# Gated attention and two expert layers: the second quarter's alpha, keys and queries loaded as rows of twelve tokens and transposed by VectorE

## The reference

```
# q, k, v, alpha: batch 2, 8 heads, 768 tokens, 48 columns
for t in range(S):
    state = alpha[:, :, t, :, None] * state + einsum('bhd,bhde', k[:, :, t], v[:, :, t])
    y[:, :, t] = einsum('bhd,bhde->bhe', q[:, :, t], state)
# x = y as 1536 tokens x 384
xn = x / sqrt(mean(x*x) + 1e-6) * rms_g
x  = (silu(xn @ w_gate) * (xn @ w_val)) @ w_out            # 384 -> 1536 -> 384
p  = probs / (sum(probs) + 1e-9)                           # 4 experts
out = sum_e p[:, e] * (relu(x @ w1[e]) @ w2[e])            # 384 -> 1024 -> 384
```

## Time and profile before

| | |
|---|---|
| time, three runs | 682.52, 683.29, 683.31 us; median 683.29 |
| the profiled execution | time 682.79 us, span 681.1 us |
| TensorE busy | 673.6 us, 99% |
| VectorE, GpSimd, ScalarE busy | 469.8, 326.8, 266.8 us |
| granted TensorE clock, mean | 1.000 of 2.4 GHz |
| DMA | 35.67 MB, mean 52 GB/s |

### The profile page before, as it was taken

How to read it: one execution, slowest core, us unless ns; L and a number is a source line. 1 busy time by engine, 2 the same in 40 slices (tenths; PEclk the granted TensorE clock), 3 DMA queues, 4 the chain that set the end, 5 groups by cost and what they waited for, 6 DMA issues and landing times.

```text
span 681.1 us, 10689 instructions
## 1 busy us (share of the span) xinstructions
PE 673.6 (99%) x3915; PEld 625.9 (92%) x3915; DVE 469.8 (69%) x839; ACT 266.8 (39%) x485; POOL 326.8 (48%) x416
## 2 busy tenths in 40 slices
PE   8999999999999999999999999999999999999998
PEld 7799999999999999998999999999999999999997
DVE  6866648674676544029976977796778678867885
ACT  4525543233422352237533443343344344434430
POOL 3579661111111118870677448645854585468100
PEclk9999999999999999999999999999999999999999
DMA  9996465006411001000020110011011101100003
GB/s 153 175 229 159 108 94 81 10 8 88 77 34 47 1 1 47 0 24 0 10 85 2 48 46 29 20 46 48 11 37 48 47 0 47 47 24 1 24 0 140
DMA packets 91911, 35.67 MB, mean 52 GB/s; under 512 B 73552, under 2 KB 91344, under 8 KB 91856
## 3 DMA queue, kind: packets, MB, share of 16 engines
q1 hardware_dynamic: 91408, 34.96, 23.1%
q10 hardware_dynamic: 448, 0.00, 0.0%
HBM read 32.00 MB, written 2.36 MB: 50 GB/s over the span
## 4 chain that ended last, share of the span: by engine, by line
PE 91%; SPq 4%; DMA 2%; POOL 1%; issue 1%; DVE 0%; ACT 0%; POOLq 0%
PE out_ps L1467 13%; PE out_ps L1468 13%; PE out_ps L1469 13%; PE hid_ps L1460 7%; PE hid_ps L1462 7%; PE hid_ps L1461 7%; PE at_ps L1719 5%; PE at_ps L1718 5%; PE at_ps L1717 5%; SPq L492 3%; PE hid_ps L1718 2%; PE hid_ps L1719 2%; PE hid_ps L1717 2%; PE at_ps L1556 1%; PE at_ps L1596 1%; PE out_ps L1718 1%
## 5 line engine op out<-in xcount | busy, mean ns | idle before, releaser
L1343 DVE SCALAR_TENSOR_TENSOR x<-out_ps,prob,x 128x384 f32<-128x384 f32 x180 | 110.3, 613 | 57.6 <-PE out_ps L1469 57.6
L1468 PE MATMUL out_ps<-early_r,late_r 128*128 128x384 f32 x384 | 129.4, 337 | 0.0
L1469 PE MATMUL out_ps<-early_r,late_r 128*128 128x384 f32 x384 | 129.3, 337 | 0.0
L1467 PE MATMUL out_ps<-early_r,late_r 128*128 128x384 f32 x384 | 129.0, 336 | 0.0
L738 POOL TENSOR_TENSOR hid_lo<-act_sb,hid_hi 128x384 fp32r<-128x384 f32 x44 | 44.7, 1016 | 152.4 <-ACT hid_hi L965 152.4
L1015 ACT COPY late<-at_ps 128x512 f32<-128x512 f32 x105 | 61.9, 589 | 101.7 <-PE at_ps L1719 98.6
L1467 PEld LDWEIGHTS out_ps<-early_r,late_r 128*128 128x128 f32 x384 | 72.1, 188 | 6.1 <-DVE x L1343 0.2
L1468 PEld LDWEIGHTS out_ps<-early_r,late_r 128*128 128x128 f32 x384 | 72.0, 188 | 5.6
L1309 DVE TENSOR_TENSOR act_sb<-hid_ps,act_sb 128x384 f32<-128x384 f32 x48 | 26.0, 541 | 72.5 <-PE hid_ps L1462 71.9
L1469 PEld LDWEIGHTS out_ps<-early_r,late_r 128*128 128x128 f32 x384 | 72.1, 188 | 0.0
L754 POOL TENSOR_TENSOR early<-stage 128x128 f32<-128x128 f32 x15 | 7.0, 465 | 102.0 <-PE at_ps L1719 102.0
(11 more groups left out here) (300 smaller groups left out, 1607.0 us busy)
## 6 DMA issues: line engine op xcount, KB each, us to landing
stage<-in_moe_w_dram SPq DMA_DIRECT2D x32, 384.0 KB, 3.6
stage<-in_moe_w_out_dram SPq DMA_DIRECT2D x4, 576.0 KB, 5.2
out_dram<-x SPq DMA_DIRECT2D x12, 192.0 KB, 1.9
stage<-in_moe_w_gate_dram SPq DMA_DIRECT2D x8, 216.0 KB, 3.9
stage<-in_moe_w_val_dram SPq DMA_DIRECT2D x8, 216.0 KB, 4.1
v_tm<-in_v_dram SPq DMA_DIRECT2D x9, 192.0 KB, 4.1
x<-in_alpha_dram SPq DMA_DIRECT2D x6, 288.0 KB, 4.6
a_tm<-in_alpha_dram SPq DMA_DIRECT2D x31, 48.0 KB, 2.3
```

What stands on the lines that cost most here:

```text
L1343: dve.scalar_tensor_tensor(out=a, in0=part, scalar=p, in1=a, op0=ALU.mult, op1=ALU.add).then_inc(s_acc, 1)
L1467: pe.matmul(dst, ah, bh, start=first, stop=False)
L1468: pe.matmul(dst, ah, bl, start=False, stop=False)
L1469: return pe.matmul(dst, al, bh, start=False, stop=last)
```

## The change

`BY_DVE` becomes 1: quarter 1 too is transposed by VectorE, and TensorE's transposes of its alpha, keys and queries go. The data come in a third form. `load_rows` gives each of 32 partitions twelve consecutive tokens (`RUN`) of one head, 560 floats (`ROW`) starting at column 0 or 32, for four lanes (two heads of a pair, two column halves). `turned` reads from such a row twelve blocks of 32 columns with a step of 48, and `turned_to` writes the transposed blocks into the bank with a step of twelve. Alpha and keys are loaded with two DMAs for a lane (the first two pairs in the order, then the other two), queries with one. The three operand tiles become one, `qka_tm`; the rows that don't fit there go into the parts of `woh` and `wol` that GpSimd's last out piece fills, and that piece waits until they have been read.

```diff
-        BY_DVE = 2
+        BY_DVE = 1
...
+        def row_slot(which, n):
+
+            if which < 2 and n >= NP - 2:
+                return (a_rows, k_rows)[which][:, n - NP + 2, :]
+            slot = n + (6, NP, 0)[which]
+            return qka_tm[:, :, :].rearrange("p c x -> p (c x)")[:, slot * ROW:(slot + 1) * ROW]
+
+        def turned(i, which, n):
+
+            if i > 1:
+                return squares_of((a_tm, k_tm, q_tm)[which], n)
+            row = row_slot(which, n)
+            return bass.AP(row.tensor, row.offset, [list(row.ap[0]), [D, RUN], [1, SQ]])
+
+        def turned_to(i, bank):
+
+            if i > 1:
+                return bank[:, :]
+            return bank[:, :].rearrange("p (r j) -> p j r", j=RUN)
...
+            def load_rows(i, which):
+
+                b, t0 = i // QB, (i % QB) * TQ
+                src, done = ((alpha, s_qka[0]), (k, s_qka[1]), (q, s_qka[2]))[which]
+                for lane in range(LANES):
+                    base = src.offset + ((b * H + lane // 2) * S + t0) * D + lane % 2 * SQ
+                    for pairs in ((slice(0, NP),) if which == 2 else (slice(NP - 2, NP), slice(0, NP - 2))):
+                        count, first = pairs.stop - pairs.start, row_slot(which, pairs.start)
+                        home = bass.AP(first.tensor, first.offset, [list(first.ap[0]), [ROW, count], [1, ROW]])
+                        rows = bass.AP(src.tensor, base + 2 * pairs.start * S * D,
+                                       [[RUN * D, SQ], [2 * S * D, count], [1, ROW]])
+                        sp.dma_start(home[lane * SQ:(lane + 1) * SQ], rows).then_inc(done, 16)
+
...
+                if i == 2:
+                    sp.wait_ge(s_tk, NP * i)
+                    sp.wait_ge(s_tq, NP * i)
+                (load_squares if i > 1 else load_rows)(i, 0)
...
+            if PIECES[n] == ("out", NQ - 1):
+                pool.wait_ge(s_ta, 2 * NP)
+                pool.wait_ge(s_tk, 2 * NP)
...
-                    dve.transpose(banks[2][:, :], squares_of(k_tm, PAIR_ORDER[f])).then_inc(s_tk, 1)
+                    dve.transpose(turned_to(i, banks[2]), turned(i, 1, PAIR_ORDER[f])).then_inc(s_tk, 1)
...
-                    dve.transpose(banks[0][:, :], squares_of(q_tm, PAIR_ORDER[f])).then_inc(s_tq, 1)
+                    dve.transpose(turned_to(i, banks[0]), turned(i, 2, PAIR_ORDER[f])).then_inc(s_tq, 1)
...
-                        dve.transpose(banks[1][:, :], squares_of(a_tm, PAIR_ORDER[f])).then_inc(s_ta, 1)
+                        dve.transpose(turned_to(i, banks[1]), turned(i, 0, PAIR_ORDER[f])).then_inc(s_ta, 1)
...
-                    todo = {"T": ((0, a_tm, 1, s_ta), (1, k_tm, 2, s_tk))[:2 if i else 1],
-                            "TK": ((1, k_tm, 2, s_tk),), "TQ": ((2, q_tm, 0, s_tq),)}[name]
+                    which, tm, bank, done = {"T": (0, a_tm, 1, s_ta), "TK": (1, k_tm, 2, s_tk),
+                                             "TQ": (2, q_tm, 0, s_tq)}[name]
```

More of the change, by code:

```diff
@@ L74, in gated_attention_two_moe @@
         reg_a = ExitStack()
-        q_tm = sb("q_tm", [P, NCH, H * LANE], stack=reg_a)
-        k_tm = sb("k_tm", [P, NCH, H * LANE], stack=reg_a)
-        a_tm = sb("a_tm", [P, NCH, H * LANE], stack=reg_a)
+        qka_tm = sb("qka_tm", [P, 3 * NCH, H * LANE], stack=reg_a)
+        q_tm, k_tm, a_tm = [qka_tm[:, n * NCH:(n + 1) * NCH, :] for n in range(3)]
         v_tm = sb("v_tm", [P, NCH, H * D], stack=reg_a)
@@ L131, in gated_attention_two_moe @@
         wvl = sb("wvl", [P, KT, FF], F32R, reg_b)
+        SQ = 32
+        RUN = TQ // SQ
+        ROW = (RUN - 1) * D + SQ
+        OUT_AT = (FT - KT) * DM
+        assert 2 * ROW <= KT * DM and 2 * AW <= OUT_AT and 8 * ROW <= 3 * NCH * H * LANE
+        reg_w = ExitStack()
+        sb("woh_front", [P, OUT_AT], stack=reg_w)
+        a_rows = sb("a_rows", [P, 2, ROW], stack=reg_w)
+        reg_w.close()
         woh = sb("woh", [P, FT, DM], F32R, reg_b)
@@ L134, in gated_attention_two_moe @@
         half_range = sb("half_range", [P, 2, AW], stack=reg_w)
+        sb("wol_front", [P, OUT_AT - 2 * AW], stack=reg_w)
+        k_rows = sb("k_rows", [P, 2, ROW], stack=reg_w)
         reg_w.close()
-        assert 2 * AW <= FT * DM
         wol = sb("wol", [P, FT, DM], F32R, reg_b)
@@ L350, in states_before, with rows_arrived @@
             return NCH * (NP * i + f) - (1 if (i, f) == (0, NP - 1) else 0)
-        SQ = 32
         NSQ = TQ // SQ
         LANES = P // SQ
-        BY_DVE = 2
+        BY_DVE = 1
         def squares_of(t, n):
             return t[:, :, :].rearrange("p c x -> p (c x)")[:, n * TQ:(n + 1) * TQ]
-        def rows_arrived(i):
-            return 16 * (NCH * min(i + 1, BY_DVE) + LANES * NP * max(i + 1 - BY_DVE, 0))
+        def row_slot(which, n):
[12 more added lines that the diff above has]
+            return bank[:, :].rearrange("p (r j) -> p j r", j=RUN)
+        def rows_arrived(i, which):
+            return 16 * (NCH + LANES * (1 if which == 2 else 2) * min(i, 1) + LANES * NP * max(i - 1, 0))
         def state_blocks(t):
@@ L535, in next_a @@
                 sp.wait_ge(s_sqa, 2)
-                (load_squares if i >= BY_DVE else load_quarter)(i, 0)
+                if i == 2:
+                    sp.wait_ge(s_tk, NP * i)
+                    sp.wait_ge(s_tq, NP * i)
+                (load_squares if i > 1 else load_rows)(i, 0)
             def next_kq(i):
@@ L541, in next_kq @@
                     sp.wait_ge(used, NP * i)
-                    (load_squares if i >= BY_DVE else load_quarter)(i, which)
+                    (load_squares if i > 1 else load_rows)(i, which)
             def next_v(i):
@@ L1133, in scale_keys @@
                 if i >= BY_DVE:
-                    dve.wait_ge(s_qka[1], rows_arrived(i))
-                    dve.transpose(banks[2][:, :], squares_of(k_tm, PAIR_ORDER[f])).then_inc(s_tk, 1)
-                    dve.wait_ge(s_qka[2], rows_arrived(i))
+                    dve.wait_ge(s_qka[1], rows_arrived(i, 1))
+                    dve.transpose(turned_to(i, banks[2]), turned(i, 1, PAIR_ORDER[f])).then_inc(s_tk, 1)
+                    dve.wait_ge(s_qka[2], rows_arrived(i, 2))
                     wait_three(dve, s_yc, i, f, 2)
-                    dve.transpose(banks[0][:, :], squares_of(q_tm, PAIR_ORDER[f])).then_inc(s_tq, 1)
+                    dve.transpose(turned_to(i, banks[0]), turned(i, 2, PAIR_ORDER[f])).then_inc(s_tq, 1)
                 own_done()
@@ L1154, in _ @@
                     if i >= BY_DVE:
-                        dve.wait_ge(s_qka[0], rows_arrived(i))
-                        dve.transpose(banks[1][:, :], squares_of(a_tm, PAIR_ORDER[f])).then_inc(s_ta, 1)
+                        dve.wait_ge(s_qka[0], rows_arrived(i, 0))
+                        dve.transpose(turned_to(i, banks[1]), turned(i, 0, PAIR_ORDER[f])).then_inc(s_ta, 1)
                     dve.wait_ge(s_ta, u + 1)
@@ L1520, in _ @@
                 if name in ("T", "TK", "TQ"):
-                    todo = {"T": ((0, a_tm, 1, s_ta), (1, k_tm, 2, s_tk))[:2 if i else 1],
-                            "TK": ((1, k_tm, 2, s_tk),), "TQ": ((2, q_tm, 0, s_tq),)}[name]
[L1523 to L1542, removed]
+                    which, tm, bank, done = {"T": (0, a_tm, 1, s_ta), "TK": (1, k_tm, 2, s_tk),
+                                             "TQ": (2, q_tm, 0, s_tq)}[name]
+                    if f < 2:
+                        pe.wait_ge(s_half[which], 16 * NCH)
+                    else:
+                        pe.wait_ge(s_qka[which], 16 * NCH)
+                    if which == 0:
+                        wait_two(pe, s_sm, i, f, 2)
+                    if which == 1:
+                        wait_two(pe, s_st, i, f, NCH)
+                    for c in range(NCH):
+                        mm = pe.transpose(banks[bank][:, c * CH:(c + 1) * CH],
+                                          tm[:, c, n * 2 * LANE:(n + 1) * 2 * LANE], ident[:, :])
+                    mm.then_inc(done, 1)
                 elif name == "S":
```

## The result

The changed kernel takes 687.06 us (median of 5 runs, 685.92 to 690.17) against 683.29 (682.52 to 683.46) before: 3.8 us slower, ratio 1.006, 95% interval 1.0047 to 1.0072. The profiled execution took 687.06 us too, its span is 685.2, 4.1 more than before.

The account below looks back on a forecast made before the run. TensorE, working 99% of the span, was taken as the bound, set from outside by weight transfers at V of tile 3. 682.8 + 4.3 - 2.3 gave 684.8 us profiled, 685.3 against the median; range 680.2 to 687.4.

Parts of the forecast that it names:

- Transposes taken off TensorE: Second quarter: 36 transposes leave TensorE at 0.11 us each; the 21 behind V of tile 3 save 2.3 us.
- VectorE, 0.58 us for a strided transpose: VectorE's twelve new 128 x 384 transposes in the second quarter were taken to cost 0.58 us each, like dense ones.
- The rival that VectorE becomes the bound: Strided transposes of 1.16 us overrun VectorE's cover in three pairs: +2.5 us, 687.8; at 2.55 us each near 700; chance 0.06.
- Rate of the row loads: Alpha, keys and queries, 3.44 MB over 32 partitions per DMA, at 218 GB/s: 15.8 us, 5.5 more than before.
- The rival of hidden transfers: Neighbouring lanes' DMAs overlap, rate near 390 GB/s, val piece lands by 45 us: gain 3.1 us, 680.2; chance 0.37.
- no such hold: SyncE, held at the keys' DMAs before while the queue ran empty, would not be held so: 1.2 us back.
- the term +4.3: Weight pieces behind the row loads land 4.3 us later (5.5 - 1.2), so V of tile 3 starts at 56.15; chance 0.52.
- 1.2 us off for the queue that ran empty before: From 31 to 33 us only 68 GB/s moved before; that lost 1.2 us, subtracted from the 5.5 us of longer loads.
- TensorE stands in front of O of tile 1, G and V of tile 3: TensorE waits in three places: for the hidden low part, the gate low part and V's weights; some 5.5 us together.
- The clock: Rival: the clock falls to 1.2 GHz in TensorE's three waits, adding +3 to +5 us, about 689; chance 0.05.
- The sum: +4.3 (V of tile 3) - 2.3 (21 transposes behind it) = +2.0 us: 684.8 profiled, 685.3 against the median.

Follow-up runs that it names:

- The computing half alone: Against the kernel before: VectorE transposes the second quarter, but its operands are loaded as before, so values differ from the reference; 680.95 us, ratio 0.9967.
- the run with the waits filled: The changed kernel plus 18 spare matmuls before O of tile 0 and of tile 1, so TensorE works through its waits; 687.01 us, ratio 1.0054.
- the kernel with spread loads: The changed kernel with the last two pairs' alpha and keys loaded behind the val piece, queries behind the gate piece of tiles 6 to 8; 683.57 us, ratio 0.9995.

## Why the prediction was right, and where it was off

- *Transposes taken off TensorE, 0.11 us each, 2.3 us behind V of tile 3:* right. The computing half alone gains 2.3 us, and a step takes 12.98 us.
- *VectorE, 0.58 us for a strided transpose:* right, 0.58 and 0.59. The rival that VectorE becomes the bound falls. The Trainium skill's note on cachelines (SBUF — State Buffer, "Door 1") puts a penalty on accesses that go to a new line each time, and where it speaks of PSUM it names matmuls. No penalty shows here on VectorE's writes with a step of 48 bytes into PSUM.
- *Rate of the row loads, 218 GB/s:* right, 219 from 36 to 40 us, and 228 from 26 to 40 with the wide out piece among them. The rival of hidden transfers falls; its mechanism is real (wide DMAs give 679.6 against its 680.2), but these DMAs are not wide.
- *"With 512 rows for a tensor in place of 3,072 I expect no such hold":* right at the rows themselves, where SyncE is hardly held (0.43 us for most), and short of what follows. Behind them the queue is full, and SyncE is held 9.6 us at v, whose DMAs are 1,024 pieces of 192 bytes each. The val piece is issued at 48.32, 7 us later than before. v before val costs 1.4 us by the medians.
- *Gate at 45.9, val at 51.8, V of tile 3 at 56.15, which is the term +4.3:* too small. The splits begin at 48.92 and 54.37, V of tile 3 comes at 58.59, +6.7. This is the mis-sized term. It is off by 2.4 us at V of tile 3 and by 3.0 at the gate piece already, so the error lies in what delays the gate piece and not in the val piece or its late issue. The working had only the rows ahead of it and took 1.2 us off for the queue that ran empty before; it had nothing for v right behind it, which stood there before too, but in a shorter queue. With v moved behind val the gate split begins at 46.52, 0.6 us from the forecast. How the rest divides between v and the 1.2 us is open. It is not the late start of the rows in this profile (24.28 and not 22.92, since the six DMAs ahead took 4.92 us to issue): in the run with the waits filled they start at 23.33, and gate and V of tile 3 come at 48.91 and 58.78 all the same.
- *TensorE stands in front of O of tile 1, G and V of tile 3:* half right. It waits at O of tile 0 too (2.23 us), for the out piece behind the alpha rows, which I had left out, and not at G of tile 3.
- *The clock:* it fell behind two of the waits, as the rival said (0.50 from 41.5 to 44.5 us), and no cost shows: with the waits filled the time is the same.
- *The sum:* +6.7 - 2.3 = +4.4 against 4.1 in the spans and 3.8 in the medians; forecast +2.0. Right in sign and mechanism and inside the range, though near its top (687.06 of 687.4); the mis-sized term is the delay.

Open: why the executions of the kernel with spread loads lie in two groups (four from 680.9 to 682.0 at a mean clock of 1.000, eight from 683.2 to 685.2, seven of them at 0.997 or 0.998). No kernel with the whole reference was found that is faster than before beyond doubt.

## What to carry to other kernels

Take the bytes that a new layout loads and the partitions that one DMA covers together: here rows of 2,240 bytes over 32 partitions ran at 219 GB/s and over 128 at 399, and 1.9 times the bytes at the lower rate cost 6.7 us of delay against 2.3 us of TensorE work saved; at the higher rate they cost nothing. Look at what stands behind the loads in the same queue, and for how long that queue stays full; moving a load within a full queue only moves the wait, so look in the profile for the stretch where it is empty. Where narrow DMAs must be, try an order in which neighbours fill different partitions, here those under and over 64 in turn, and keep the large count in the first dimension.

## What was not expected of the hardware

- A DMA with a leading dimension of 2 ran on 2 of 16 engines, at 51 GB/s in place of some 220.
- The order of twenty narrow DMAs alone changed their rate from 219 to 286 GB/s.
- A DMA of 1,024 pieces of 192 bytes, behind a full queue, held SyncE for 3.3 and 5.8 us, where row DMAs of 2,240-byte pieces took 0.43 us for most.
